# Packed values with v as weights, reciprocals through DRAM, and a new order of attention's steps

## Chip, core, metric

One core of one Trainium2 chip. The metric is the device time of one execution in microseconds (us), median of the runs. The profiled execution is one of its own, told beside them.

## The reference

The computation is attention through packed tokens, then two feed-forward networks, all in float32:

```
q, k, v: (8 batches, 8 heads, 576, 64);  p: (8, 8, 32, 64)
packed = softmax(p k^T / 8) v                 # per batch and head: 32 x 64
out    = softmax(q packed^T / 8) packed       # 576 x 64
x      = out as 4608 tokens x 512
x      = x / sqrt(mean(x^2) + 1e-6) * rms_g
x      = (silu(x w_gate) * (x w_val)) w_out   # 512 -> 1536 -> 512
h      = x w_in                               # 512 -> 2048
y      = (max(h, 0) + alpha * min(h, 0)) w_out2
```

Each softmax subtracts its row's maximum and adds 1e-9 to the sum of its exponentials.

## The kernel before

**Stages.** A prologue does batch 0's attention. Then come eight tiles, one for each batch's 576 tokens, in `tiles_of_a`; a tile has 24 blocks (`up_block`), each the gate and the value product of 128 hidden units and 288 tokens: 2 x 2 x 3 matmuls of 128x128 weights and 288 columns, "three passes" of float32 split in a high and a low part (L883 to L885). ScalarE takes the silu of the gate (L1373), VectorE the product with the value part (L1748). After the tiles, from about 423 us on apart from the last tile's blocks, come the wide products (`PHASES`); the change does not touch them.

**Attention beside the tiles.** While tile c - 1 runs, batch c's attention is done in its gaps ("batch c's share" below). Dictionaries give, for each engine, the names of the steps that stand at a place of a tile: `("within", i)` after the gate's part of block i (on VectorE and ScalarE: before their work on block i), `("ready", i)` before the last three matmuls of block i, `("after", i)` and then `("between", i)` behind it. `SECOND` holds batch 1's steps, `LATER` those of batches 2 to 7; `NEXT` the first steps of the batch behind (scores, maxima, exponentials, keys), `CARRIED` the last ones of the batch ahead (fold4, fold5). At one place, carried steps stand first, then the batch's own, then those of the next. The order on each engine is fixed by this; semaphores order the engines.

**The steps of a batch.** `scores` (p against k), their maxima and `exp`; `turn_keys`: VectorE transposes the exponentials in 32x32 blocks to `a_rows`, SP writes them to DRAM (`a_mid`) and `turned_keys` reads them back with keys in partitions (`a_keys`). `packed`: TensorE multiplies exponentials (weights, 128x32) by v (64 columns moving), VectorE scales rows by the reciprocal sums into `pp`, `turn_packed` transposes it on TensorE, ScalarE copies it to `pp_t`, and VectorE's `scaled` makes `pp_tg` (times `rms_g`). `tokens0/1`: scores of the 576 tokens against the packs, and the packs' own products. VectorE then works through `turn_s`, `max2`, `shift`, `sums`, `probs`, `turn_p` with ScalarE's exponentials between; `gram0/1` multiply the token weights by the packs' own products (`gram_sb`, 32x32 for each head), `weigh` and `means` give each token's mean square, `rsqrt` on ScalarE and `newton` on VectorE its inverse root, `normed` and `split` the scaled weights in two parts (`an_hi`, `an_lo`). `fold0` to `fold5` multiply the packed values by the gate and value weights (L1087), ScalarE casts the high part and VectorE subtracts the low part (`m_hi`, `m_lo`); these are the weights of the batch's tile.

**Waits that matter.** Block i's gate product may start when silu i - 2 is done, its value product when VectorE's product i - 2 is done (the two pairs of PSUM banks alternate). ScalarE loads a function table when it goes from silu to exponentials and back. `q_sb` lies on `k_sb`, so k of the next batch is loaded when this batch's tokens are done. SP's queue is in order: at each block stores of hidden units, moves of weight parts that GpSimd prepares in this stage, loads, and the two parts of `turn_keys`.

Of the kernel before, what the change touches and what calls it, by code (L numbers as in the profile page):

```python
# [7 lines left out]
F32 = mybir.dt.float32  # L8
# [5 lines left out]
P = 128  # L14
BATCH, HEADS, SEQ, HEAD_DIM = 8, 8, 576, 64
PACK = 32
# [49 lines left out]
           ("ready", 22): ["fold2_ready"], ("after", 22): ["fold2"],  # L66
# [8 lines left out]
            ("after", 20): ["newton"], ("within", 21): ["normed0"], ("after", 21): ["normed1", "fold1"],  # L75
            ("after", 22): ["split0"], ("within", 23): ["split1"], ("after", 23): ["fold2"],
            ("between", 23): ["fold3"]},
# [4 lines left out]
                   ("within", 22): ["split0"], ("after", 22): ["split1"], ("after", 23): ["fold2"], ("between", 23): ["fold3"]},  # L82
}
LATER = {
    "PE": {("between", 0): ["packed"], ("within", 2): ["turn_packed"],
           ("ready", 3): ["tokens0_ready"], ("after", 3): ["tokens0", "tokens1_ready", "tokens1"],
           ("between", 11): ["gram0", "fold0_ready", "fold0"],
           ("between", 13): ["gram1", "fold1_ready", "fold1"],
           ("between", 16): ["means", "fold2_ready", "fold2"],
           ("ready", 20): ["fold3_ready"], ("after", 20): ["fold3"]},  # L90
    "DVE": {("after", 0): ["norm0", "norm1", "packed"], ("after", 2): ["scaled"],
            ("after", 3): ["turn_s0", "gram"], ("after", 4): ["turn_s1", "max2_0"],
            ("after", 5): ["shift0", "max2_1"], ("within", 6): ["shift1"],
            ("between", 7): ["sums0"], ("after", 8): ["probs0"], ("after", 9): ["turn_p0", "sums1"],
            ("within", 10): ["probs1"], ("after", 10): ["turn_p1"],
            ("after", 11): ["weigh0"], ("after", 12): ["fold0"],
            ("after", 14): ["weigh1"], ("after", 15): ["fold1"],
            ("after", 17): ["newton"], ("after", 18): ["normed0"], ("after", 19): ["normed1", "fold2"],
            ("after", 20): ["split0"], ("after", 21): ["split1"], ("after", 22): ["fold3"]},
    "Activation": {("after", 2): ["packed"], ("after", 6): ["probs0", "probs1", "silu"], ("after", 12): ["fold0"],  # L100
                   ("after", 14): ["fold1"], ("after", 16): ["rsqrt"], ("after", 18): ["fold2"], ("after", 19): ["split0"],
# [4 lines left out]
    "DVE": {("between", 11): ["max0"], ("between", 13): ["max1"], ("between", 15): ["turn_keys"]},  # L106
# [87 lines left out]
def build(nc, q_t, k_t, v_s, p_t, w1_gv, w_parts, rms_g, alpha, out_t):  # L194
# [8 lines left out]
    with ExitStack() as ctx:  # L203
# [174 lines left out]
        def at_ps(c, t):  # L378
# [1633 lines left out]
```

## Time and profile before

| | |
|---|---|
| median of 3 runs | 1419.37 us (1418.79 to 1419.72) |
| profiled execution | 1417.08 us, span 1415.3 us |
| TensorE busy | 1391.8 us, 98% of the span |
| VectorE, ScalarE, GpSimd busy | 1067.0 (75%), 762.0 (54%), 271.1 us (19%) |
| granted TensorE clock | 0.999 of 2.4 GHz |
| busy share of the DMA engines | 80% |

"Busy" is the union of an engine's instructions. For TensorE their ends are modelled and overlap the next start, so short waits hide in it; the starts in the timeline tell more. Times in rows are from the span's start.

### The profile page before, as it was taken

The page shows a single profiled execution, that of the slowest core. Times are in us where ns is not written, and L with a number is a line of the kernel's source. Part 1 is how long each engine was busy: PE and PEld are TensorE (multiplying, and loading weights), DVE is VectorE, ACT ScalarE, POOL GpSimd, SP SyncE. Part 2 cuts the span into 40 slices and gives each one's busy share as a digit, 9 for nine tenths or more (in the row PEclk, how much of TensorE's full clock was granted, in tenths as well). Part 3 has the DMA queues.
Part 4 walks back from the last instruction along what each step waited for, and adds up shares of the span by engine and source line. Part 5 has one row for each costly group of instructions (what it writes and reads, how often), then busy time and mean ns, then how long its engine had stood idle before and what let it go on. Part 6 is the DMA issues. An engine that isn't in the chain of part 4 may idle for free.

```text
span 1415.3 us, 24525 instructions
## 1 busy us (share of the span) xinstructions
PE 1391.8 (98%) x9318; PEld 1194.7 (84%) x9318; DVE 1067.0 (75%) x1669; ACT 762.0 (54%) x1241; POOL 271.1 (19%) x464
## 2 busy tenths in 40 slices
PE   8999999999999999999999999999999999999998
PEld 4767787877879888888888888899888899999998
DVE  5767767777675689578987578986788876886786
ACT  4556466455543546356655356553566554664564
POOL 1744665666872000000000000000000000000000
PEclk9999999999999999999999999999999999999999
DMA  9768978979869987768797658798669788798775
GB/s 344 228 205 282 316 262 287 312 271 293 279 215 369 341 309 246 227 207 290 293 301 240 228 183 325 254 315 277 199 216 331 243 299 306 259 333 278 251 264 189
DMA packets 152372, 384.47 MB, mean 272 GB/s; under 512 B 9920, under 2 KB 66752, under 8 KB 143296
## 3 DMA queue, kind: packets, MB, share of 16 engines
q1 hardware_dynamic: 152112, 382.84, 80.0%
q8 instruction: 74, 1.21, 0.3%
q14 instruction: 42, 0.34, 0.1%
q10 hardware_dynamic: 144, 0.07, 0.0%
HBM read 286.27 MB, written 87.16 MB: 264 GB/s over the span
## 4 chain that ended last, share of the span: by engine, by line
PE 86%; DVE 5%; DMA 4%; ACT 3%; issue 2%; SPq 1%; POOL 0%; DVEq 0%; ACTq 0%; POOLq 0%
PE psum L883 27%; PE psum L884 27%; PE psum L885 27%; DMA k_sb<-k_t 3%; PE psum L1087 2%; PE psum L1028 1%; DVE act_sb L1748 1%; DMA g_sb<-rms_g 1%; PE psum L962 1%; PE psum L1049 0%; DVE m_lo L1690 0%; DVE sq L1657 0%; DVE sq L1654 0%; SPq L570 0%; ACT L1373 0%
## 5 line engine op out<-in xcount | busy, mean ns | idle before, releaser
L883 PE MATMUL psum<-stage_hi,ring 128*128 128x512 f32 (+1 forms) x980 | 360.3, 368 | 0.4
L885 PE MATMUL psum<-stage_lo,ring 128*128 128x512 f32 (+1 forms) x980 | 359.9, 367 | 0.0
L884 PE MATMUL psum<-stage_hi,ring 128*128 128x512 f32 (+1 forms) x980 | 359.9, 367 | 0.0
L1389 ACT CAST stage_hi<-g_sb 128x512 fp32r<-128x512 f32 (+1 forms) x384 | 221.9, 581 | 201.2 <-PE psum L885 198.6
L1767 DVE TENSOR_TENSOR stage_lo<-g_sb,stage_hi 128x512 fp32r<-128x512 f32 (+1 forms) x384 | 240.9, 638 | 67.4 <-ACT stage_hi L1389 66.6
L883 PE MATMUL psum<-an_hi,m_hi 128*128 128x288 f32 x768 | 236.0, 307 | 11.6 <-DVE act_sb L1748 5.9
L884 PE MATMUL psum<-an_hi,m_lo 128*128 128x288 f32 x768 | 226.1, 294 | 0.0
L885 PE MATMUL psum<-an_lo,m_hi 128*128 128x288 f32 x768 | 226.0, 294 | 0.0
L885 PE MATMUL psum<-x_lo,ring_up 128*128 128x512 f32 (+1 forms) x560 | 205.6, 367 | 0.0
L884 PE MATMUL psum<-x_hi,ring_up 128*128 128x512 f32 (+1 forms) x560 | 205.6, 367 | 0.0
L883 PE MATMUL psum<-x_hi,ring_up 128*128 128x512 f32 (+1 forms) x560 | 205.6, 367 | 0.0
L883 PEld LDWEIGHTS psum<-stage_hi,ring 128*128 128x128 f32 x980 | 184.0, 188 | 24.8 <-DVE stage_lo L1767 1.4
L885 PEld LDWEIGHTS psum<-stage_lo,ring 128*128 128x128 f32 x980 | 184.0, 188 | 22.9
L884 PEld LDWEIGHTS psum<-stage_hi,ring 128*128 128x128 f32 x980 | 184.0, 188 | 22.8
L883 PEld LDWEIGHTS psum<-an_hi,m_hi 128*128 128x128 f32 x768 | 144.2, 188 | 58.2 <-issue 33.0
L1748 DVE TENSOR_TENSOR act_sb<-act_sb,psum 128x288 f32<-128x288 f32 x192 | 85.6, 446 | 112.1 <-PE psum L885 60.0
L1373 ACT ACTIVATE act_sb<-psum 128x288 f32<-128x288 f32 x192 | 78.3, 413 | 152.4 <-PE psum L885 152.1
L884 PEld LDWEIGHTS psum<-an_hi,m_lo 128*128 128x128 f32 x768 | 144.6, 188 | 0.1
L885 PEld LDWEIGHTS psum<-an_lo,m_hi 128*128 128x128 f32 x768 | 144.4, 188 | 0.0
L885 PEld LDWEIGHTS psum<-x_lo,ring_up 128*128 128x128 f32 x560 | 105.1, 188 | 13.2
L883 PEld LDWEIGHTS psum<-x_hi,ring_up 128*128 128x128 f32 x560 | 105.1, 188 | 13.1
L884 PEld LDWEIGHTS psum<-x_hi,ring_up 128*128 128x128 f32 x560 | 105.1, 188 | 13.0
(152 smaller groups left out, 1775.2 us busy)
## 6 DMA issues: line engine op xcount, KB each, us to landing
ring<-w_down SPq DMA_DIRECT2D x70, 1024.0 KB, 5.2
ring<-w_out SPq DMA_DIRECT2D x70, 768.0 KB, 5.8
ring_up<-w_up SPq DMA_DIRECT2D x40, 1024.0 KB, 5.3
ring_up<-w_up SPq DMA_DIRECT2D x40, 768.0 KB, 4.6
h_mid<-act_sb SPq DMA_DIRECT2D x84, 288.0 KB, 4.2
g_sb<-h_mid SPq DMA_DIRECT2D x10, 1536.0 KB, 10.5
w_up<-parts SPq DMA_DIRECT2D x16, 896.0 KB, 5.9
w_down<-parts SPq DMA_DIRECT2D x16, 896.0 KB, 6.0
```

Of the source, the lines that this page charges most:

```text
L883: nc.tensor.matmul(dst, w_hi, hi, start=start, stop=False, skip_group_check=onto)
L884: nc.tensor.matmul(dst, w_lo, hi, start=False, stop=False, skip_group_check=onto)
L885: return nc.tensor.matmul(dst, w_hi, lo, start=False, stop=stop, skip_group_check=onto)
L962: mm = nc.tensor.matmul(pp_ps(c, e)[PACK * pair:PACK * (pair + 1), :], a_keys[:, e * PAIRS + pair, j, :], v_sb[:, j, head * HEAD_DIM:(head ...
L1028: mm = nc.tensor.matmul(psum[keys, gram_bank(c, h) + e, 0:HALF], gram_sb[keys, e, :], a2[keys, h, e, :], start=True, stop=True)
L1087: mm = nc.tensor.matmul(psum[keys, m_bank(c, j) + e, :].rearrange("p (f n) -> p f n", f=2), pp_tg[c % 2][dims, pair, :], gv_sb[dims, 2 * j ...
L1373: nc.scalar.activation(dst, gate_ps(n), ACT.Silu).then_inc(silu_done, 1)
L1389: nc.scalar.copy(stage_hi[:, n % STAGES, 0:w], block_of(k, ROLE[i], j)).then_inc(stage_hi_done, 1)
L1748: nc.vector.tensor_tensor(dst, dst, val_ps(n), ALU.mult).then_inc(h32_done, 1)
L1767: nc.vector.tensor_tensor(stage_lo[:, n % STAGES, 0:w], block_of(k, ROLE[i], j), stage_hi[:, n % STAGES, 0:w].bitcast(F32), ALU.subtract). ...
```

## The change

For batches 2 to 7, v's 64 dims of a head become the weights (128x64) and the exponentials move (32 columns), two heads side by side. The packed values come out turned, so `turn_packed` and ScalarE's copy go. The scaling must then be along columns: the reciprocal sums are written to DRAM and read back as a row for each pair, broadcast over 64 partitions (`rcp_rows`), and VectorE multiplies once. For all batches `gram_sb` becomes 128x128, zero outside the four heads' blocks by a mask (`own`) that GpSimd sets at the start, and `gram` is one matmul instead of four for each of its two halves. Many steps move by a block, k's load stands before and v's behind a part's moves, and some batches get dictionaries of their own.

```diff
@@ SECOND, batch 1 (only what changes) @@
-           ("ready", 22): ["fold2_ready"], ("after", 22): ["fold2"],
+           ("ready", 21): ["fold2_ready"], ("after", 21): ["fold2"],
...
-            ("after", 20): ["newton"], ("within", 21): ["normed0"], ("after", 21): ["normed1", "fold1"],
-            ("after", 22): ["split0"], ("within", 23): ["split1"], ("after", 23): ["fold2"],
-            ("between", 23): ["fold3"]},
+            ("within", 20): ["newton"], ("after", 20): ["normed0"], ("within", 21): ["normed1"], ("after", 21): ["fold1"],
+            ("within", 22): ["split0"], ("after", 22): ["split1", "fold2"], ("after", 23): ["fold3"]},
...
-                   ("within", 22): ["split0"], ("after", 22): ["split1"], ("after", 23): ["fold2"], ("between", 23): ["fold3"]},
+                   ("within", 21): ["split0"], ("after", 21): ["split1"], ("after", 22): ["fold2"], ("after", 23): ["fold3"]},
 LATER = {
-    "PE": {("between", 0): ["packed"], ("within", 2): ["turn_packed"],
+    "PE": {("between", 0): ["packed"],
            ("ready", 3): ["tokens0_ready"], ("after", 3): ["tokens0", "tokens1_ready", "tokens1"],
-           ("between", 11): ["gram0", "fold0_ready", "fold0"],
-           ("between", 13): ["gram1", "fold1_ready", "fold1"],
-           ("between", 16): ["means", "fold2_ready", "fold2"],
-           ("ready", 20): ["fold3_ready"], ("after", 20): ["fold3"]},
-    "DVE": {("after", 0): ["norm0", "norm1", "packed"], ("after", 2): ["scaled"],
+           ("between", 12): ["gram0", "fold0_ready", "fold0"],
+           ("between", 14): ["gram1", "fold1_ready", "fold1"],
+           ("between", 17): ["means", "fold2_ready", "fold2"],
+           ("between", 19): ["fold3_ready", "fold3"]},
+    "DVE": {("after", 0): ["packed", "scaled"],
             ("after", 3): ["turn_s0", "gram"], ("after", 4): ["turn_s1", "max2_0"],
             ("after", 5): ["shift0", "max2_1"], ("within", 6): ["shift1"],
-            ("between", 7): ["sums0"], ("after", 8): ["probs0"], ("after", 9): ["turn_p0", "sums1"],
-            ("within", 10): ["probs1"], ("after", 10): ["turn_p1"],
-            ("after", 11): ["weigh0"], ("after", 12): ["fold0"],
-            ("after", 14): ["weigh1"], ("after", 15): ["fold1"],
-            ("after", 17): ["newton"], ("after", 18): ["normed0"], ("after", 19): ["normed1", "fold2"],
+            ("between", 8): ["sums0"], ("after", 9): ["probs0"], ("after", 10): ["turn_p0", "sums1"],
+            ("within", 11): ["probs1"], ("after", 11): ["turn_p1"],
+            ("after", 12): ["weigh0"], ("after", 13): ["fold0"],
+            ("between", 15): ["fold1"], ("after", 15): ["weigh1"],
+            ("within", 18): ["newton"], ("after", 18): ["normed0"], ("after", 19): ["normed1", "fold2"],
             ("after", 20): ["split0"], ("after", 21): ["split1"], ("after", 22): ["fold3"]},
-    "Activation": {("after", 2): ["packed"], ("after", 6): ["probs0", "probs1", "silu"], ("after", 12): ["fold0"],
-                   ("after", 14): ["fold1"], ("after", 16): ["rsqrt"], ("after", 18): ["fold2"], ("after", 19): ["split0"],
+    "Activation": {("after", 7): ["probs0", "probs1", "silu"], ("after", 13): ["fold0"],
+                   ("after", 15): ["fold1"], ("after", 17): ["rsqrt"], ("after", 18): ["fold2"], ("after", 19): ["split0"],
                    ("after", 20): ["split1"], ("after", 21): ["fold3"]},
 }
...
-    "DVE": {("between", 11): ["max0"], ("between", 13): ["max1"], ("between", 15): ["turn_keys"]},
+    "DVE": {("between", 11): ["max0"], ("between", 13): ["max1"], ("between", 15): ["norm0", "norm1", "turn_keys"]},
...
+LAST_BATCH = {**LATER, "Activation": {**LATER["Activation"], ("after", 6): ["probs0", "probs1", "silu"], ("after", 7): []}}
+
+CARRIED_FIRST = {
+    "PE": {("ready", 6): ["fold4_ready", "fold5_ready"], ("after", 6): ["fold4", "fold5"]},
+    "DVE": {("between", 6): ["fold4"], ("after", 7): ["fold5"]},
+    "Activation": {("after", 6): ["fold4"], ("after", 7): ["fold5"]},
+}
+CARRIED_LAST = {
+    "PE": {("ready", 0): ["fold4_ready"], ("after", 0): ["fold4"], ("ready", 7): ["fold5_ready"], ("after", 7): ["fold5"]},
+    "DVE": {("after", 1): ["fold4"], ("after", 8): ["fold5"]},
+    "Activation": {("after", 1): ["fold4"], ("after", 8): ["fold5"]},
 }
...
-            return [4, 6, 4, 2, 6, 4][j] if first(c) else ([6, 6, 2, 6, 6, 6] if c == 1 else [6, 6, 6, 2, 6, 6])[j]
+            return [4, 6, 4, 2, 6, 4][j] if first(c) else ([6, 6, 2, 6, 6, 2] if c == 1 else [6, 6, 6, 2, 6, 6])[j]
...
             def turn_keys(c):
+                sp.wait_ge(rcp1_done, GROUPS * (c + 1))
+                reached(sp, rcp_in, 32 * (c - 2))
+                for g in range(GROUPS):
+                    sp.dma_start(rcp_mid[g].unsqueeze(1), rcp1[:, g:g + 1]).then_inc(rcp_out, 16)
                 for g in range(GROUPS):
                     sp.wait_ge(rows_turned, GROUPS * (c - 2) + g + 1)
                     sp.dma_start(a_mid[g], a_rows[:, g, :]).then_inc(rows_out, 16)
 
             def turned_keys(c):
                 sp.wait_ge(pp_mm, 2 * c)
+                sp.wait_ge(rcp_out, 16 * GROUPS * (c - 1))
+                sp.wait_ge(ppt_copied, c)
+                for e in range(2):
+                    sp.dma_start(rcp_rows[HEAD_DIM * e:HEAD_DIM * (e + 1)].rearrange("p q k -> p (q k)"),
+                                 rcp_mid[e].partition_broadcast(HEAD_DIM)).then_inc(rcp_in, 16)
                 sp.wait_ge(rows_out, 16 * GROUPS * (c - 1))
...
-                    if c + 1 < BATCH and i == (8 if c == 1 else 2):
+                    if c + 1 < BATCH and i == (8 if c == 1 else 7):
                         sp.wait_ge(pp_mm, 2 * c + 2)
                         load_v(c + 1)
-                    if c + 1 < BATCH and i == (10 if c == 1 else 4):
+                    if c + 1 < BATCH and i == (10 if c == 1 else 3):
...
+            nc.gpsimd.memset(own[:], 0.0).then_inc(zeroed, 1)
+            for pair in range(PAIRS):
+                pool.wait_ge(zeroed, pair + 2)
+                nc.gpsimd.memset(own[PACK * pair:PACK * (pair + 1), pair, :], 1.0).then_inc(zeroed, 1)
+            pool.wait_ge(zeroed, PAIRS + 2)
...
-                for e in range(2):
+                for pair in range(PAIRS):
                     for j in range(CHUNKS):
-                        for pair in range(PAIRS):
+                        for e in range(2):
                             head = 2 * pair + e
-                            mm = nc.tensor.matmul(pp_ps(c, e)[PACK * pair:PACK * (pair + 1), :],
+                            mm = nc.tensor.matmul(ppt_of(e)[:, PACK * pair:PACK * (pair + 1)],
+                                                  v_sb[:, j, head * HEAD_DIM:(head + 1) * HEAD_DIM],
                                                   a_keys[:, e * PAIRS + pair, j, :],
-                                                  v_sb[:, j, head * HEAD_DIM:(head + 1) * HEAD_DIM],
                                                   start=(j == 0), stop=(j == CHUNKS - 1))
-                    mm.then_inc(pp_mm, 1)
+                mm.then_inc(pp_mm, 2)
 
...
-                    for pair in range(PAIRS):
-                        keys = slice(PACK * pair, PACK * (pair + 1))
-                        mm = nc.tensor.matmul(psum[keys, gram_bank(c, h) + e, 0:HALF], gram_sb[keys, e, :], a2[keys, h, e, :],
-                                              start=True, stop=True)
+                    mm = nc.tensor.matmul(psum[:, gram_bank(c, h) + e, 0:HALF], gram_sb[:, e, :], a2[:, h, e, :],
+                                          start=True, stop=True)
...
             def norm(c, g):
 
                 n = GROUPS * c + g + 1
+                if g == 0:
+                    reached(dve, rcp_out, 16 * GROUPS * (c - 2))
                 dve.wait_ge(exp1_done, n)
...
             def packed(c):
+                if c > 1:
+                    dve.wait_ge(rcp_in, 32 * (c - 1))
+                    dve.wait_ge(pp_mm, 2 * c + 2)
+                    nc.vector.tensor_tensor(flat(pp_t[:]), psum[:, 3, 0:P], flat(rcp_rows[:]), ALU.mult).then_inc(ppt_copied, 1)
+                    return
                 reached(dve, ppt_mm, c)
                 dve.wait_ge(rcp1_done, 2 * c + 2)
                 for e in range(2):
             def scaled(c):
                 dve.wait_ge(ppt_copied, c + 1)
                 reached(dve, m_mm, NF1 // 2 * (c - 1))
-                nc.vector.tensor_tensor(pp_tg[c % 2][:], ppt_ps.rearrange("p (q k) -> p q k", q=PAIRS),
+                turned = pp_t[:] if c > 1 else ppt_ps.rearrange("p (q k) -> p q k", q=PAIRS)
+                nc.vector.tensor_tensor(pp_tg[c % 2][:], turned,
                                         g_sb[:].unsqueeze(2).to_broadcast([P, PAIRS, PACK]), ALU.mult).then_inc(ppg_done, 1)
 
...
-                bank, at = (4, 0) if first(c) else (2, HALF)
-                nc.vector.tensor_copy(gram_sb[:], psum[:, bank:bank + 2, at:at + PACK]).then_inc(gram_set, 2)
+                for e in range(2):
+                    within = own_ps(c, e).unsqueeze(1).to_broadcast([P, PAIRS, PACK])
+                    nc.vector.tensor_tensor(gram_sb[:, e, :].rearrange("p (q k) -> p q k", q=PAIRS), within, own[:],
+                                            ALU.mult).then_inc(gram_set, 1)
```

`CARRIED` itself stays; `SECOND`'s ScalarE steps split0 to fold3 come a block earlier. The new buffers are `own`, `rcp_rows` and `rcp_mid` (DRAM); `rinv_0` and `mean_0` move onto `a_keys`.

## Rows read from the trace of the kernel before

**Rows 1.** Who TensorE waited for, 97.5 to 423 us: idle in total, times, longest.

```profile
PE psum L883 <- DVE act_sb L1748: 4.6, 7, 1.6
PE psum L883 <- DMA k_sb<-k_t: 1.3, 3, 0.6
PE psum L1087 <- DVE m_lo L1690: 0.9, 2, 0.6
PE psum L883 <- DVE m_lo L1690: 0.7, 2, 0.3
PE psum L912 <- DMA k_sb<-k_t: 0.4, 2, 0.2
```

**Rows 2.** Timeline of TensorE, batch 5: start, duration, line, operands; packed step and transpose.

```profile
260.24 1.32 PE L962 MATMUL psum<-v_sb,a_keys 128*32 128x64 f32 x80
261.49 0.40 PE L883 MATMUL psum<-an_hi,m_hi 128*128 128x288 f32 x1
261.73 0.29 PE L884 MATMUL psum<-an_hi,m_lo 128*128 128x288 f32 x1
...
263.83 0.29 PE L885 MATMUL psum<-an_lo,m_hi 128*128 128x288 f32 x1
...
264.21 0.29 PE L884 MATMUL psum<-an_hi,m_lo 128*128 128x288 f32 x1
```

**Rows 3.** Timeline of TensorE, batch 5: a wait, gram0 and the means.

```profile
278.00 0.29 PE L885 MATMUL psum<-an_lo,m_hi 128*128 128x288 f32 x1
278.63 0.37 PE L883 MATMUL psum<-an_hi,m_hi 128*128 128x288 f32 x1 [0.34 <-DVE m_lo L1690]
...
284.03 1.17 PE L1028 MATMUL psum<-a,gram_sb 32*32 32x288 f32 x16
285.13 1.09 PE L1087 MATMUL psum<-gv_sb,pp_tg 64*32 64x512 f32 x16
...
296.47 1.13 PE L1049 MATMUL psum<-sq,mean_w 128*128 128x288 f32 x4
297.53 1.09 PE L1087 MATMUL psum<-gv_sb,pp_tg 64*32 64x512 f32 x16
```

**Rows 4.** Weight loads by shape, 97.5 to 423 us: busy us, mean ns.

```profile
L884 PEld LDWEIGHTS psum<-an_hi,m_lo 128*128 128x128 f32 x576 | 108.2, 188 | 0.0
...
L962 PEld LDWEIGHTS psum<-v_sb,a_keys 128*32 128x32 f32 x480 | 7.0, 110 | 5.0 <-issue 5.0
```

**Rows 5.** Timeline of ScalarE, batch 5: table, exponentials, silu, casts.

```profile
272.41 1.28 ACT L1290 ACT_TABLE_LOAD   x1
273.70 1.26 ACT L1292 ACTIVATE e<-e 128x576 f32<-128x576 f32 x2
...
276.28 0.41 ACT L1373 ACTIVATE act_sb<-psum 128x288 f32<-128x288 f32 x1
276.58 1.07 ACT L1335 CAST m_hi<-psum 128x512 fp32r<-128x512 f32 x2
...
290.55 0.77 ACT L1269 ACTIVATE a_sb<-a_sb,bias 128x576 f32<-128x576 f32 x1
```

**Rows 6.** Timeline of VectorE: row sums' start and second bias, batches 5 and 6.

```profile
278.40 0.74 DVE L1593 TENSOR_REDUCE sum<-e 128x18 f32<-128x576 f32 x1
...
290.93 0.15 DVE L1523 TENSOR_SCALAR bias<-negmax 128x1 f32<-128x1 f32 x1
...
332.46 0.74 DVE L1593 TENSOR_REDUCE sum<-e 128x18 f32<-128x576 f32 x1
...
345.94 0.15 DVE L1523 TENSOR_SCALAR bias<-negmax 128x1 f32<-128x1 f32 x1
```

**Rows 7.** Instructions on `a_keys`: first and last start; transfers' time to landing.

```profile
L962 PE MATMUL psum<-v_sb,a_keys x480: 218/219/244, 97.5 to 370.6; 128*32 128x64 f32 x160
L597 SPq DMA_DIRECT2D a_keys<-a_mid x24: 360/529/1384, 89.5 to 360.6; - x24
...
DMA to landing us min/median/max: 3.1/4.6/5.4
```

More of the change, by code:

```diff
@@ L111 @@
            ("ready", 15): ["scores1_ready"], ("after", 15): ["scores1"]},
-    "DVE": {("between", 16): ["max0", "max1"], ("between", 19): ["turn_keys"]},
+    "DVE": {("between", 16): ["max0", "max1"], ("between", 19): ["norm0", "norm1", "turn_keys"]},
     "Activation": {("after", 14): ["scores0"], ("between", 15): ["scores1"], ("after", 17): ["exp0", "exp1", "silu"]},
@@ L198, in build @@
     a_mid = nc.dram_tensor("a_mid", (GROUPS, P, SEQ), F32, kind="Internal").ap()
+    rcp_mid = nc.dram_tensor("rcp_mid", (GROUPS, P), F32, kind="Internal").ap()
     w_out = nc.dram_tensor("w_out", (PRODUCTS, P, DUOS1, 2, 2, P), F32, kind="Internal").ap()
@@ L250, in build @@
         a2 = place("a2", [P, 2, GROUPS, HALF])
-        gram_sb = place("gram_sb", [P, 2, PACK])
+        gram_sb = place("gram_sb", [P, 2, P])
+        own = place("own", [P, PAIRS, PACK])
         p_sb = place("p_sb", [P, PAIRS, PACK])
@@ L275, in build @@
         a_sb = place("a_sb", [P, GROUPS, SEQ])
+        a_keys_at = cursor[0]
         a_keys = place("a_keys", [P, HEADS, CHUNKS, PACK])
-        rinv_0, mean_0 = place("rinv_0", [P, 2, HALF]), place("mean_0", [P, 2, HALF])
-        assert gv_at + 4 * NF1 * KC * GV <= g_at + 4 * FIRST_CHUNK * 4 * WMAX and cursor[0] >= t3_at
+        assert gv_at + 4 * NF1 * KC * GV <= g_at + 4 * FIRST_CHUNK * 4 * WMAX
+        cursor[0] = max(cursor[0], t3_at)
         pp_tg = [place(f"pp_tg{n}", [P, PAIRS, PACK]) for n in range(2)]
+        rcp_rows = place("rcp_rows", [P, PAIRS, PACK])
+        rinv_0 = place("rinv_0", [P, 2, HALF], at=a_keys_at)
+        mean_0 = place("mean_0", [P, 2, HALF], at=a_keys_at + 2 * step)
         part_size, source_size = 4 * PRODUCTS * 2 * P, 4 * 4 * P
@@ L376, in pp_ps, with ppt_of @@
             return psum[:, e, 0:HEAD_DIM] if first(c) else psum[:, 3, e * HEAD_DIM:(e + 1) * HEAD_DIM]
+        def ppt_of(e):
+            return psum[HEAD_DIM * e:HEAD_DIM * (e + 1), 3, 0:P]
         def at_ps(c, t):
@@ L535, in at @@
                     place = (where, i)
-                    for name in (starting if c == 1 else CARRIED[name_of]).get(place, []):
+                    carried = (starting if c == 1 else CARRIED_FIRST[name_of] if c == 2 else
+                               CARRIED_LAST[name_of] if c == BATCH - 1 else CARRIED[name_of])
+                    for name in carried.get(place, []):
                         beside(c - 1, name)
                     if c < BATCH:
-                        for name in (SECOND if c == 1 else LATER)[name_of].get(place, []):
+                        steps = SECOND if c == 1 else LAST_BATCH if c == BATCH - 1 else LATER
+                        for name in steps[name_of].get(place, []):
                             beside(c, name)
@@ L982, in tokens_ready @@
                 else:
[L983 removed]
+                    pe.wait_ge(m_lo_done, evicted(c - 1) + 2 * (4 if c == 2 else 5))
             def tokens(c, h):
@@ L1072, in fold_ready @@
                     pe.wait_ge(m_lo_done, evicted(c) + 2 * 2)
+                elif j == 4 and c == 1:
+                    pe.wait_ge(s2_turned, 4 * (c + 1) + 4)
+                elif j == 5 and c == 1:
+                    pe.wait_ge(s2_turned, 4 * (c + 1) + 2)
+                    pe.wait_ge(gram_set, 2 * (c + 1) + 2)
                 elif j == 5 and c + 1 < BATCH:
```

3 lines of the change are left out of this document (2 added, 1 removed).

## Prediction

> **What bounds the kernel now.** I read the page first. TensorE counts as busy 98% of the span (the table ahead), so a stretch of the kernel costs what TensorE's own instructions cost there plus what it waits. The change touches only the stage with attention, to about 423 us; everything after it is left as it is.
>
> Busy time hides things here: a matmul's modelled end overlaps the next start. So I read starts. In batch 5's share of the stage (its packed step begins at 260.24, batch 6's at 314.29) 18 matmuls of the first matrix product lie between 261.49 and 263.83, 0.13 us each; a block of 12 is 1.58 us. Returning from small matmuls costs 0.11 more (261.49 to 261.73 is 0.24), and about 0.1 on the way out [rows 2].
>
> Then I read who makes TensorE wait. From 97.5 to 423 us it waits 16 times, 7.9 us by the view [rows 1]. By starts each is about 0.16 longer: at 278.00 the next start comes 0.63 later, 0.50 over the usual 0.13, where the view has 0.34 [rows 3]. That makes 7.9 + 16 x 0.16 = 10.5 us in six batches. Seven, 4.6 us, are for the product of block 18 or of another late block (L1748), held up by VectorE; the others are for k's transfer and for `m_lo`.
>
> **The change, part by part.** Times are against the profiled execution (1417.08 us, span 1415.3).
>
> *Packed values with v as weights.* Before: 40 calls, 80 instructions, weights 128x32 and 64 columns moving, four column tiles at once: 1.25 us to the next block [rows 2], or (1.25 - 0.11)/20 = 0.057 us for each four. After: 80 instructions with weights 128x64 and 32 columns moving, two tiles at once. Twice as many steps, 40. By the columns that move, each could take half: no change. By the weights, which are now twice as wide, it takes what their load takes. A load of 128 columns takes 188 ns and one of 32 takes 110 [rows 4]: 0.81 ns a column, so 64 columns stream in 52 ns (an estimate from the two rows). 40 x 0.052 + 0.11 = 2.19 us. That is +0.94 us, six times: **+5.6**. Bounds: 0 (loads hidden) and +12 (load and stream one after the other in each tile, 40 x (0.052 + 0.027) + 0.11 = 3.3). I take the load because 52 ns is above what 32 moving columns need (half of the 0.057 step) and the old step, where the load's 26 ns lay below, showed no sign of it.
>
> The Trainium skill, "TensorEngine Tiling (Array Packing)", section "Instruction Overhead", says that a matmul pays some 60 cycles, so that few moving columns cost as much as 60. By it 64 and 32 columns would cost alike, and this part would be 0; its 80 x 25 ns = 2.0 us (an estimate from the page) is contradicted by the 1.25 us for 80 instructions here.
>
> *No transpose of the packed values.* At 263.83 to 264.21 three starts take 0.38 instead of 0.26 [rows 2]: -0.12, six times: **-0.7**. ScalarE's copy and two VectorE scalings go, one VectorE product comes; none of them is waited for by TensorE.
>
> *Token weights as two full matmuls.* 1.10 us for 16 small ones (284.03 to 285.13) against 1.06 for the two full-size f32 calls of the means (296.47 to 297.53) [rows 3]: -0.04, some 15 times: **-0.6**. The masked copy is two VectorE products instead of one copy, some 0.3 us more. In batches 1 to 7 that lies in VectorE's idle time behind the transposes; in batch 0 the chain has no cover: **+0.3**. GpSimd's five small memsets end before the first data come.
>
> *Newton's step before block 18's product.* Now block 17's silu stands behind ScalarE's means chain, VectorE waits for it, then does Newton's three operations, then block 18's product, and block 20 waits. After the change the means stand after block 17, block 17's product is free of that chain, and fold3 (1.02 us) stands before block 20. Newton can start at the end of ScalarE's exponential, some 6.9 us after the means' start, and takes 2.3; block 20's second half starts 2 us later than that needs. So those waits go. k's load is issued ahead of a part's store and of v, so its waits go too, and m_lo's with it, since fold5's casts now stand ahead of the exponentials' table. I take all 16 as gone: **-10.5**.
>
> *What is late next.* Two things.
> (a) The exponentials now stand behind block 7's silu and behind fold5's two casts. From silu 7's start ScalarE does: 0.30 to the casts, casts 1.07, table 1.28, exponentials 1.26, table 1.28, silu 8 0.41 [rows 5], with gaps and the hand-over 5.7. Silu 7 starts 0.2 behind its gate. TensorE has from there: half a block 0.79, blocks 8 and 9 3.16, the scores' four passes (as the means', 1.06, plus 0.2) = 5.2. Block 10 needs silu 8: it waits 5.9 - 5.2 = 0.7 us, in the five batches that have scores: **+3.5**. Before, the exponentials stood one block earlier and the casts behind them.
> (b) With silu 8 late, VectorE's row sums ("between 8", behind block 8's product) start with block 10 at the earliest. From the sums to the second bias VectorE works without a pause: 278.40 to 291.08 = 12.7 us, and 13.6 in batch 6 [rows 6]; over the five batches 12.5 to 13.6, mean 12.9. The new order has the same work in that stretch. Behind the bias ScalarE needs the exponential (0.77 and its sum's read, 0.86), a table 1.28 and silu 14 0.41 [rows 5], together 2.65. TensorE needs silu 14 for block 16: six blocks 9.5 and two pairs of gram and fold (2 x (1.06 + 1.02 + 0.2)) after block 10's start, 14.1. Wait: 12.9 + 2.65 - 14.1 = 1.4 us, five times: **+7.1** (fold1's wait for fold0's `m_lo` is part of it). Bounds: 0 and 2.2 each.
>
> *Batch 1's end.* Newton, normed and fold2 come a block earlier and fold4 leaves the place before the packed step. That step began at 97.5 [rows 7] and could come at 93, but it needs the keys, whose transfers were issued from 89.5 and take up to 5.4 us to land, about 95 [rows 7]. Their issue can come 1 us earlier (block 21's product is earlier) and two more issues stand before them, so the keys still land at about 95. Gain 97.5 - 95.0 - 1.0 for fold4, which now follows: **-1.5** (bounds -3 and 0).
>
> *Reciprocals through DRAM.* Two writes of 128 values and two broadcasts, on SP's queue. At `i == 15` SP waits for VectorE's transposed rows in any case; the new wait for `rcp1_done` is earlier, since the norms stand directly before. Behind SP there stand block 15's store and a part's moves, which wait today too. The broadcasts stand before the four key transfers: they delay these, which take 4.6 us to land by the median [rows 7], by about 1, with some 2 us left before the packed step. **0** (without that cover, 1 us six times).
>
> Sum: 5.6 - 0.7 - 0.6 + 0.3 - 10.5 + 3.5 + 7.1 - 1.5 = +3.2, on a profiled 1417.1. The median of the runs shown is 2.3 above that execution; added to the median: 1419.4 + 3.2 = **1422.6 us**. What can be told from no change here is 0.2%, 2.8 us.
>
> **Rivals.**
> 1. *The packed step costs what it cost*, because weights are loaded behind the other tile's stream. For it: nothing in the old step shows a load. Against: 52 ns is longer than the stream. 1422.6 - 5.6 = 1417.0: within 0.2%. Chance 0.20.
> 2. *The two late silus don't stop TensorE* (faster). Place: blocks 10 and 16. It decides if silu 8 comes 0.7 us and silu 14 1.4 us sooner than I count, say if VectorE's chain is shorter because its long operations (1.4 us instead of 0.75 for one product of the same size) fall elsewhere. Against: the sequence on ScalarE is fixed and every length in it is steady. 1422.6 - 10.6 = 1412.0. Chance 0.23, since half of it would do for "faster" together with a cheaper packed step.
> 3. *Load and stream don't overlap within a tile.* 6 x (3.3 - 2.19) = 6.7 more: 1429.3. Against: the old step's 0.057 is less than 26 + 53. Chance 0.10. The Trainium skill, "TensorE: Matmul & The Clock Gate", section "The mechanism", says that a load overlaps a running matmul only where the row group differs, and both tiles here hold all rows; the old step, which is of the same kind, contradicts it by the sum just given.
> 4. *The keys are late* behind the reciprocals' transfers, in every batch: from 2 us on it decides; 1 us six times gives 1428.6. For it: the queue's work is in order. Chance 0.05.
>
> **How the numbers follow.** Forecast 0.42, its own range 1419.5 to 1427. It lies just over the 0.2% line (1422.2): about 0.33 of it slower, 0.09 same. Slower 0.33 + 0.10 + 0.05 less a little for batch 1's bound = 0.46; faster 0.23 and a few hundredths of rival 1 = 0.26; same 0.28. The range reaches from just above rival 2's full size to short of rival 3: 1412.5 to 1427.5.
>
> **What would show it.** The packed step (start of its first instruction to the next block's) at 2.2 us; no transpose behind it; no wait before block 20; in batches 2 to 6 a wait at block 10 that ScalarE's silu ends, about 0.7, and one at block 16, about 1.4, or at fold1 for `m_lo`; batch 5's period 1.3 longer than its 54.05 us; batch 7's some 1.7 shorter; the packed step of batch 2 near 95. Wrong it would be with a packed step of 1.3 or of 3.3, or with blocks 10 and 16 starting on time.

## The result, and the profile after

The changed kernel takes **1460.03 us** (median of 5 runs, 1458.47 to 1462.7), the kernel before 1419.72 us in the same comparison (1418.79 to 1420.55): ratio 1.0284, interval 1.027 to 1.0298. The forecast was 1422.6 with a range to 1427.5. The side was right, the size was not: 40 us instead of 3. The profiled execution has a span of 1458.2 us (before 1415.3), TensorE busy 1405.2 us, and a granted clock of 0.987.

The first view is again who TensorE waits for, from 97.5 us to the end of the tiles (engine, line <- what it waited for: us in total, times, longest):

```profile
PE psum L1002 <- DMA a_keys<-a_mid: 30.5, 6, 7.1
PE psum L923 <- ACT act_sb L1416: 7.0, 10, 0.8
PE psum L1130 <- DVE m_lo L1743: 0.5, 1, 0.5
PE psum L923 <- DVE act_sb L1801: 0.2, 1, 0.2
```

The waits of [rows 1] have gone almost all, as forecast. The ten for silu are (a) and (b) of the prediction. The first line is new: the packed step (L1002) waits for its keys in all six batches. The timeline of TensorE in batch 5 shows what such a wait does (start, duration, line, operands):

```profile
283.50 1.09 PE L1130 MATMUL psum<-gv_sb,pp_tg 64*32 64x512 f32 x16
289.59 4.48 PE L1002 MATMUL psum<-a_keys,v_sb 128*64 128x32 f32 x80 [5.00 <-DMA a_keys<-a_mid]
294.00 0.55 PE L923 MATMUL psum<-an_hi,m_hi 128*128 128x288 f32 x1
294.39 0.30 PE L924 MATMUL psum<-an_hi,m_lo 128*128 128x288 f32 x1
```

From the step's start to the next block are 4.41 us, against 1.25 in [rows 2] and 2.19 forecast. The table by windows explains it (start:end, length, busy us and instructions of PE, PEld, DVE, ACT and POOL, granted clock, DMA share, GB/s):

```profile
281.00:284.00 3.00, 3.00 (x36) 2.51 (x34) 1.87 (x4) 0.82 (x2) 0.00 (x0) 1.00 1.00 406
284.60:289.50 4.90, 0.00 (x0) 0.00 (x0) 0.00 (x0) 0.00 (x0) 2.85 (x7) 0.80 1.16 295
289.60:293.90 4.30, 4.30 (x80) 4.30 (x80) 0.00 (x0) 0.00 (x0) 3.21 (x6) 0.50 1.04 417
294.50:298.00 3.50, 3.50 (x29) 3.50 (x28) 2.33 (x5) 1.79 (x4) 3.44 (x7) 1.00 0.48 189
```

TensorE stood idle for 5 us, the granted clock fell in that time from 1.00 to 0.50 (2.4 to 1.2 GHz), and the whole packed step ran at the lower level.

Why the keys are late stands in SP's waits (97.5 to 505) and in its timeline:

```profile
SPq L617 <- DVE rcp L1578: 38.0, 5, 8.2
SPq L625 <- DMA rcp_mid<-rcp: 22.3, 5, 5.6
```

```profile
269.51 0.80 SPq L617 DMA_DIRECT2D rcp_mid<-rcp  x2
270.35 0.90 SPq L620 DMA_DIRECT2D a_mid<-a_rows  x2
...
279.19 2.39 SPq L627 DMA_DIRECT2D rcp_rows<-rcp_mid  x2
281.62 2.08 SPq L632 DMA_DIRECT2D a_keys<-a_mid  x4
```

The wait at L617 is for VectorE and harmless: SP has arrived early. The one at L625 isn't: SP stands until 1 KB of reciprocals, issued at 269.5, is in DRAM, and goes on at 279.2. The keys are issued at 281.6, 11.3 us behind the rows. The transfers of that stretch (269.5 to 281; the digits are the busy share of the 16 DMA engines in 40 equal slices, below them the GB/s moved):

```profile
DMA  0002207999999090013969999219990176921099
GB/s 0 0 0 2 2 0 305 385 385 369 321 16 16 0 8 0 0 8 24 32 24 40 24 56 16 16 16 97 40 32 16 16 24 72 88 16 24 16 361 483
```

From the twelfth slice to the 38th (272.7 to 280.4) the DMA engines are busy half of the time (5.1 tenths, the mean of the digits) and move 27 GB/s (mean of the figures), where just before and after that they move 300 to 480. Busy share without throughput: something is stuck in front.

### The profile page after: what moved, and what is told of

The parts are those of the page before. It is cut to its first block, busy times and chain, and to the rows that moved or that the text cites. A ratio compares the mean times of both kernels' runs of the same rounds, so it can differ in the third digit from the quotient of the medians.

```text
span 1458.2 us, 24157 instructions
## 1 busy us (share of the span) xinstructions
PE 1405.2 (96%) x9120; PEld 1217.8 (84%) x9120; DVE 1065.1 (73%) x1671; ACT 760.1 (52%) x1235; POOL 261.6 (18%) x469
## 4 chain that ended last, share of the span: by engine, by line
PE 80%; DVE 7%; DMA 7%; ACT 3%; issue 2%; SPq 1%; POOL 0%; DVEq 0%; ACTq 0%; POOLq 0%
PE psum L923 25%; PE psum L924 25%; PE psum L925 25%; DMA a_keys<-a_mid 2%; DMA a_mid<-a_rows 2%; DMA rcp_mid<-rcp 2%; PE psum L1002 2%; PE psum L1130 1%; DVE act_sb L1801 1%; DVE m_lo L1743 1%; ACT L1405 1%; SPq L632 1%; DVE sq L1684 1%; PE psum L1032 0%; DVE a L1662 0%
## 5 line engine op out<-in xcount | busy, mean ns | idle before, releaser
L923 PE MATMUL psum<-an_hi,m_hi 128*128 128x288 f32 x768 | 235.6, 307 | 10.6 <-ACT act_sb L1416 7.9
## 6 DMA issues: line engine op xcount, KB each, us to landing
g_sb<-h_mid SPq DMA_DIRECT2D x10, 1536.0 KB, 10.5
```

Of the source, the lines that this page charges most:

```text
L923: nc.tensor.matmul(dst, w_hi, hi, start=start, stop=False, skip_group_check=onto)
```

## The experiments

### First: which part of the change costs what

**The new order alone** (old packed step, reciprocals used in SBUF as before, full-size token weights kept):

```diff
@@ in words @@
-    a_keys moving, v as weights; rcp_mid written and read; L1002's loop
+    v moving, a_keys as weights, turn_packed, scaling of rows: as in the kernel before
```

> The new order and the full-size gram stay, packed values and reciprocals are as before the change (exponentials as weights, transpose, two scalings, no transfer of reciprocals). Theory 1 (the loss is the packed step, 6 x 3.2 = 19 us, and the waits for the keys behind the reciprocals' transfers, 6 x 5 = 30 us; the order by itself gains): 1460 - 49 = about 1411, faster than before by 8. Theory 2 (the new order, with v's load behind, makes the keys late): still waits of about 5 us before the packed step, about 1441.

Measured 1412.66 us (1411.27 to 1413.16), ratio 0.9938, interval 0.9916 to 0.9961. The packed step is back to 1.25 us and its keys are late once, by 1.1. So the new order is a gain of 8.8 us by the medians (5.8 us by the profiled executions), and the whole loss of the change lies in the packed step and the way of its inputs.

**The new packed step, reciprocals kept in SBUF.** VectorE scales the exponentials' rows before it transposes them; nothing goes through DRAM that did not before:

```diff
+    nc.vector.tensor_scalar(a_sb[:, g, :], a_sb[:, g, :], rcp1[:, g:g + 1], None, ALU.mult)
     nc.vector.transpose(a_rows[:, g, :], a_sb[:, g, :])
-    sp.dma_start(rcp_mid...), sp.dma_start(rcp_rows...)
```

> As after the change, but VectorE scales the exponentials by the reciprocal sums before it transposes them (two more operations of 128x576 a batch), and no reciprocal goes through DRAM. Theory 1: the keys land some 9 us after the rows' store instead of 19, no wait before the packed step, the packed step stays at 4.4 us: 1460 - 30 = about 1430. Theory 2: waits stay, 1455 or more.

Measured 1422.38 us (1421.24 to 1423.52), ratio 1.0007, interval 0.9994 to 1.002: no difference from before that can be told. I had expected some 1430, with a packed step that stays at 4.4 us. It doesn't: with its inputs in time it runs at the full clock and takes 2.46 us in all six batches:

```profile
264.54 2.52 PE L993 MATMUL psum<-a_keys,v_sb 128*64 128x32 f32 x80
266.99 0.40 PE L914 MATMUL psum<-an_hi,m_hi 128*128 128x288 f32 x1
```

That is +1.21 each and +7.3 in all; with 3.5 us more waits for VectorE's products, and 0.7 less for the transposes that are gone, it is 10.1, and the medians are 9.7 us over the order alone.

**Rows and keys ahead of the reciprocals** in SP's queue, all else as in the changed kernel:

```diff
@@ in words @@
+    rows' write, then the reciprocals' write; keys' read, then the reciprocals' read
-    the other way round
```

> As after the change, but the rows' store is issued ahead of the reciprocals' write, and the keys' load ahead of the reciprocals' read. If what costs is only that rows and keys stand behind the small transfers in the queue: no wait before the packed step, about 1430. If the small writes hold up all that shares the 16 engines, wherever they stand: the keys are still late, or VectorE's product waits for the reciprocals, and the time stays over 1440.

Measured 1455.99 us (1454.76 to 1461.46), ratio 1.0249, interval 1.0222 to 1.0277. The keys are as late as before (30.1 us in all). The rows, now in front, land 2.3 us after their issue by the median, though single ones still take up to 11. But the keys' transfers, issued from 209.6 in batch 4 while SP need not wait for the reciprocals, take 12 to 13 us to land (6.6 by the median of all batches, 4.5 in the order alone). The place in front isn't enough: what is issued behind the reciprocals' write is slow.

**Both moves added to the kernel before**, with their result unused:

```diff
+    sp.dma_start(rcp_mid[g].unsqueeze(1), rcp1[:, g:g + 1])       # ahead of the rows
+    sp.dma_start(rcp_rows[...], rcp_mid[e].partition_broadcast(HEAD_DIM))  # ahead of the keys
```

> The kernel before, with the reciprocals' write and read added at the same places of SP's queue (and the norms moved ahead of the keys' transposes); nobody uses what is read. Theory 1: the keys land some 8 us later than before, the packed step waits about 4 us in each of six batches: about 1443. Theory 2: within 0.3% of before.

Measured 1439.17 us (1438.59 to 1441.04), ratio 1.0126, interval 1.0106 to 1.0146: about 18 us of the loss, in the old order too. The keys there are late by 15.4 us in all.

### Second: the write or the read, the bytes or the place

All of these but the last stand on the new order alone (1412.7 us), and nobody reads the values.

**The write alone, and the same with each value 512 bytes from the next:**

```diff
+    sp.dma_start(rcp_mid[g].unsqueeze(1), rcp1[:, g:g + 1])      # rcp_mid (2, 128)
```
```diff
+    sp.dma_start(rcp_mid[g, :, 0:1], rcp1[:, g:g + 1])           # rcp_mid (2, 128, 128)
```

> The new order with the old packed step (1412.7 us), and only the two writes of 128 reciprocals of 4 bytes, which nobody reads. Theory W (the writes themselves hold the transfer queue): the rows behind them land some 10 us after their issue instead of 2.1, the keys' issue waits for that, the packed step waits 3 to 5 us in five or six batches at once with a fall of the clock: 1430 to 1440. Theory R (the broadcasts hold it): 1412 to 1415 and rows that land in 2 to 3 us.

> As the run before, but every one of the 256 values goes to an address 512 bytes from the next. If the writes are slow because all of them fall into the same few hundred bytes of DRAM, the rows land in 2 to 4 us and the time is 1412 to 1416. If they are slow because each is a transfer of 4 bytes, nothing changes against the run before (1430 to 1440).

The write alone: 1443.31 us (1442.3 to 1446.47), ratio 1.017, interval 1.0154 to 1.0186. It costs 30.6 us. That is somewhat above the 1430 to 1440 expected. The same 256 values of 4 bytes, spread: 1411.54 us (1410.94 to 1412.41), ratio 0.9943, interval 0.9928 to 0.9957: nothing. SP's timeline, first side by side, then apart:

```profile
198.77 0.79 SPq L617 DMA_DIRECT2D rcp_mid<-rcp  x2
199.61 0.91 SPq L620 DMA_DIRECT2D a_mid<-a_rows  x2
209.62 1.89 SPq L627 DMA_DIRECT2D a_keys<-a_mid  x4
```

```profile
188.63 0.80 SPq L617 DMA_DIRECT2D rcp_mid<-rcp  x2
189.47 0.91 SPq L620 DMA_DIRECT2D a_mid<-a_rows  x2
193.53 3.29 SPq L627 DMA_DIRECT2D a_keys<-a_mid  x4
```

The issues of writes and rows cost SP the same. From the rows' issue to the keys' are 10 us against 4.1. Side by side, SP stands there until the rows are in DRAM, as its waits say; apart, that line is gone, the writes land in 1.5 us by the median and the rows in 2.5:

```profile
SPq L624 <- DMA a_mid<-a_rows: 27.2, 5, 6.3
```

**The read alone** (the write made for batch 2 only):

```diff
+    if c == 2: sp.dma_start(rcp_mid[g].unsqueeze(1), rcp1[:, g:g + 1])
+    sp.dma_start(rcp_rows[...], rcp_mid[e].partition_broadcast(HEAD_DIM))   # every batch
```

> As the first, but the reciprocals are written for batch 2 alone and the two broadcasts over 64 partitions are made in every batch (unused). Theory W: the keys land 1 to 2 us later than in the new order alone, about 6.5 us after their issue, and the packed step waits little: 1413 to 1420. Theory R: 1430 to 1440.

Measured 1419.0 us (1417.44 to 1423.47), ratio 1.0005, interval 0.9992 to 1.0017. The only late keys are batch 2's, behind the one write, by 5.1 us, and there the packed step runs at half clock (2.29 us), as does the block behind it until 103.6. Wait, step and block account for the 6.3 us over the order alone. From batch 3 on the broadcasts cost TensorE nothing: the packed step starts on time.

**The changed kernel, reciprocals turned first.** VectorE transposes them in 32x32 blocks, so that a write is 4 runs of 128 bytes:

```diff
+    nc.vector.tensor_copy(rcp_wide[:, 0:GROUPS], rcp1[:])
+    nc.vector.transpose(rcp_turned[:], rcp_wide[:])
-    sp.dma_start(rcp_mid[g].unsqueeze(1), rcp1[:, g:g + 1])
+    sp.dma_start(rcp_mid[g].rearrange("(q k) -> q k", k=PACK), rcp_turned[g:P:PACK, :])
```

> The changed kernel with one thing different: VectorE turns the reciprocals in 32x32 blocks first, so each write is 4 runs of 128 bytes instead of 128 values of 4 bytes. If the number of small pieces holds the queue, the writes and the rows land in 2 to 3 us, the keys are late by 0 to 1 us a batch, the packed step takes 2.46 us at the full clock, and the time is 1418 to 1425 (1422.4 with the reciprocals kept in SBUF, less 4 us of VectorE waits there). If any extra transfer and its wait in SP's queue is enough, the keys still wait 4 to 5 us a batch: 1450 to 1460.

Measured 1420.95 us (1418.95 to 1424.56), ratio 1.0008, interval 0.9996 to 1.002. With the same waits, the same queue and the same bytes, 39 of the 40 us are gone. The packed step takes 2.46 us, and only batch 2's keys are late, by 2.3.

### Third: the packed step, and the silu waits

**Three forms of the packed step** on the kernel with reciprocals kept in SBUF (one execution each, read from the traces): the five calls of a head in a row instead of alternating between the heads; each moving column given twice; and 32 dims as weights in four column tiles.

```diff
-    for j in range(CHUNKS):
-        for e in range(2):
+    for e in range(2):
+        for j in range(CHUNKS):
```
```diff
-    a_keys[:, e * PAIRS + pair, j, :]
+    a_keys[:, e * PAIRS + pair, j, :].unsqueeze(1).to_broadcast([P, 2, PACK])
```
```diff
-    for e in range(2):      # weights v_sb[:, j, 64 dims of head 2 * pair + e]
+    for n in range(4):      # weights v_sb[:, j, 32 dims], output psum[32 * n:32 * (n + 1)]
```

> The changed kernel with reciprocals kept in SBUF (its packed step took 2.46 us at the full clock), the five calls of one head one after the other instead of alternating between the two halves of TensorE's columns. If the overlap needs neighbours in different halves the step takes 3.5 to 4.8 us, otherwise 2.46.

> As the run before in its base, with every one of the 32 moving columns given twice, so 64 columns move past the same weights. If the weights' load sets the step (my forecast: two halves side by side, 59 ns a pair of instructions) it stays 2.46 us. If load and stream lie one behind the other in each half (old step 57 ns for 32 + 64 columns, new step 59 ns for 64 + 32: 0.6 ns a column), it takes 40 x 0.078 + 0.11 = 3.2 us.

> The same base with 32 of a head's dims as weights in each call, four column tiles side by side, 160 instructions instead of 80. Load alone: 40 x 0.026 + 0.11 = 1.15 us; load and stream one after the other: 40 x 0.038 + 0.11 = 1.65 us; if each instruction costs what it costs now (31 ns) however narrow it is: 4.9 us.

In that order, the step and the block behind it:

```profile
266.81 3.41 PE L993 MATMUL psum<-a_keys,v_sb 128*64 128x32 f32 x80
270.15 0.40 PE L914 MATMUL psum<-an_hi,m_hi 128*128 128x288 f32 x1
```
```profile
263.22 2.55 PE L994 MATMUL psum<-a_keys,v_sb 128*64 128x64 f32 x80
265.71 0.40 PE L914 MATMUL psum<-an_hi,m_hi 128*128 128x288 f32 x1
```
```profile
266.38 1.56 PE L993 MATMUL psum<-a_keys,v_sb 128*32 128x32 f32 x160
267.88 0.40 PE L914 MATMUL psum<-an_hi,m_hi 128*128 128x288 f32 x1
```

The executions took 1427.65, 1423.07 and 1438.31 us. Start to start the steps take 3.33, 2.48 and 1.49 us; only the second is one of the values expected. Less the 0.11 for the switch and divided by the rounds (one instruction in each tile that runs side by side), weights x moving columns:

| form | tiles | rounds | ns a round |
|---|---|---|---|
| before: 32 x 64 | 4 | 20 | 57 |
| changed: 64 x 32 | 2 | 40 | 59 |
| moving columns doubled: 64 x 64 | 2 | 40 | 59 |
| 32 x 32 | 4 | 40 | 34.5 |

Twice the moving columns cost nothing, half the weights' width saves 24 ns. In these four forms, whose neighbouring instructions go to different tiles, a round takes what the wider of load and stream takes, about 0.9 ns a column at 64. That the sum of both counts is refuted by the third line (78 ns expected, 59 measured). The form with a head's calls in a row has 40 ns an instruction against 29.5 in the alternating one. It doesn't follow from this reading as it stands: a tile that takes 59 ns for its load would take 59, not 40, unless the other tile's instructions still ran beside it for part of the time. The runs don't tell which, so the reading is shown for the alternating forms alone.

The third form's step is 0.97 us shorter than its base's, yet its execution is 16 us longer: TensorE has five waits in it, 15.0 us in all, that no semaphore ends:

```profile
PE psum L914 <- issue: 6.9, 2, 4.4
PE psum L916 <- issue: 4.4, 2, 3.0
PE psum L993 <- issue: 3.7, 1, 3.7
```

The edit adds 80 matmul instructions to a batch, and as many weight loads. The DMA view has a queue of the kind "instruction", which brings pieces of 16 KB. Each of the five waits has just one such piece in it or at its start, and TensorE goes on 1.4 to 1.6 us after the piece has ended. For the longest wait, the view from 331 to 332.2 and the end of the wait:

```profile
q8 instruction: 1, 0.02, 5.0%
```
```profile
333.55 0.61 PE L914 MATMUL psum<-an_hi,m_hi 128*128 128x288 f32 x1 [4.42 <-issue]
```

So TensorE most likely ran out of instructions behind a step that uses them up in 1.5 us. This is read from the trace; no run varied it.

**The token exponentials a block earlier**, on the new order alone:

```diff
-    "Activation": {..., ("after", 7): ["probs0", "probs1", "silu"]
+    "Activation": {..., ("after", 6): ["probs0", "probs1", "silu"]
```

> The new order with the old packed step (1412.7 us), with the token exponentials of batches 2 to 7 back behind block 6's silu. My theory: both waits of TensorE for silu (blocks 10 and 16, 0.8 us each, 7.2 in all) come from the exponentials' late place; they go, and the time is 1412.7 - 7 = 1405 to 1407. The rival: the old place brings back the waits that the old order had (for m_lo and VectorE's products), and the time is 1410 to 1414.

Measured 1409.16 us (1408.46 to 1409.72), ratio 0.992, interval 0.9906 to 0.9934: the lowest median of all versions. It gains 3.5 us over the order alone by the medians and 2.1 by the profiled spans (1409.5 and 1407.4), where I expected some 7. The two intervals (to 0.9934, and from 0.9916) overlap a little. Its waits:

```profile
PE psum L914 <- ACT act_sb L1407: 2.9, 4, 1.3
PE psum L914 <- DVE m_lo L1726: 1.9, 5, 0.4
PE psum L993 <- DMA a_keys<-a_mid: 1.0, 1, 1.0
```

Silu's waits fall from 7.2 us (ten) to 2.9 (four), and five for `m_lo` appear, 1.9 us (the kernel before had four, 1.6 us; the order alone has one, 0.8): both theories have a part.

### Fourth: how near, and two terms of the sum

**The unused write with 64, and with 16 bytes between the values** (one execution each):

```diff
-    rcp_mid (GROUPS, P, P)
+    rcp_mid (GROUPS, P, 16)        # and in the other run (GROUPS, P, 4)
```

> The new order with the unused write of the reciprocals, each value 64 bytes from the next (at 4 bytes apart: rows land 9 us after their issue, 1443; at 512 apart: 2.2 us, 1411.5). If small writes are held up only when they fall in one piece of 64 bytes or less, this is as at 512: rows in 2.2 us, 1410 to 1413. If the piece is 512 bytes: between the two, rows in 3 to 9 us, 1415 to 1443.

> As the run before with 16 bytes between the values. If writes within 64 bytes of each other hold each other up, four values share a piece instead of 16: the writes still take a good part of their 7 us, rows in 3 to 7 us, 1412 to 1435. If the piece is 16 bytes or less, 1410 to 1413.

1411.01 and 1412.29 us. The rows' time to landing, first at 64 bytes, then at 16 (minimum, median, maximum; at 512 it was 2.2/2.5/4.8):

```profile
DMA to landing us min/median/max: 2.2/2.5/5.8
```
```profile
DMA to landing us min/median/max: 3.1/3.3/6.5
```

At 64 bytes there is nothing left of the effect; at 16, four values to each 64 bytes, the rows are 0.8 us later; at 4 bytes, sixteen to each, they land 9 to 10 us after their issue. The cost grows with the number of small writes that fall close together. At 16 it came out at the lower end of what I had expected.

**Small token weights again**, on the new order alone:

```diff
-    gram_sb (128, 2, 128), one matmul a half, masked by own
+    gram_sb (128, 2, 32), four matmuls a half, one copy
```

> The new order (1412.7 us) with the packs' own products as four small matmuls a half and one copy, as before. By my terms (-0.6 and +0.3 for the full-size version) this is 0.3 us slower: 1412.5 to 1413.5. If the mask on VectorE costs anything in batches 1 to 7, it is faster by 1 or more: 1409 to 1412.

Measured 1412.48 us (1412.1 to 1414.04), ratio 0.9953, interval 0.994 to 0.9967, against 0.9938 (0.9916 to 0.9961) with the full-size ones. The intervals overlap: that part of the change is worth nothing that can be told.

**VectorE's sums and probabilities a block earlier too:**

```diff
-    ("between", 8): ["sums0"], ("after", 9): ["probs0"], ("after", 10): ["turn_p0", "sums1"], ("within", 11): ["probs1"], ("after", 11): ["turn_p1"]
+    ("between", 7): ["sums0"], ("after", 8): ["probs0"], ("after", 9): ["turn_p0", "sums1"], ("within", 10): ["probs1"], ("after", 10): ["turn_p1"]
```

> As the run with the token exponentials a block earlier (1409.2 us), and VectorE's sums, probabilities and transposes a block earlier too, where they stood before. VectorE then fills the 1.3 us that it is idle in block 9, its second maximum comes earlier, and block 16's wait for the silu (2.9 us over four places) goes: 1405 to 1407. Rival: the sums now stand in front of a product that TensorE waits for, and the time is 1409 to 1413.

Measured 1415.46 us (1414.23 to 1417.4), ratio 0.9975, interval 0.9966 to 0.9984: 6.3 slower than without it, and above both values expected. The waits for silu fall to 1.6 us, but the sums now stand in front of products that TensorE needs:

```profile
PE psum L914 <- DVE act_sb L1784: 4.1, 6, 1.7
PE psum L914 <- DVE m_lo L1726: 2.1, 5, 0.4
PE psum L914 <- ACT act_sb L1407: 1.6, 2, 1.3
```

With the 1.2 us for batch 2's keys, TensorE waits some 3 us longer here than in the version before, and the profiled spans (1413.0 and 1407.4) are 5.6 apart: the rest isn't placed.

## Why the prediction was wrong

**The step that failed** is "Reciprocals through DRAM ... 0". It gave the two writes no time of their own, and looked for cover at the broadcasts. The write costs 30.6 us by itself; the read costs nothing once the write is out of the way, and in the changed kernel 39 of the 40 us go when the write leaves in runs. The sentence "the new wait for `rcp1_done` is earlier" looked at the wrong wait: not the one for the values to be ready, but those for values and rows to be in DRAM (L625 and the one ahead of L632), which hold SP's queue. In batch 5 the keys are issued 11.3 us behind the rows; in the new order alone it is 5.1. Slack was about what was said: 2.9 us there between the keys' landing (254.8) and the packed step (257.7). With it used up, the wait is 5.0. Rival 4 named the place and the sign, and set its price at 1 us a batch and its chance at 0.05: the old trace has no transfer of 4-byte pieces, and the prediction went by large ones, without a bound for pieces some 500 times smaller. Its condition, "from 2 us on it decides", was met in every batch.

**What was missing altogether** is the clock. A late input was priced at its lateness. The six waits are 29.7 us longer by starts than in the new order alone (33.7 against 4.0, from the start before the packed step to its own). The packed steps add 17.8 more: 25.3 us in the six batches against 7.5, of which 7.3 are their price at the full clock and 10.5 the halved one. 29.7 + 17.8 = 47.5. The profiled spans are 48.7 apart (the medians 47.4): the blocks right behind the steps, whose starts are 0.24 us apart instead of 0.13 until the clock is back, add some 2, and the transposes that are gone take 0.7 off. The Trainium skill, "TensorE: Matmul & The Clock Gate", section "HAM oscillation — how this bites in real kernels", describes a clock that falls while TensorE waits for DMA, so that the next work starts at the lower level; the windows above agree (1.00 to 0.50 in 5 us of idle time).

**The side was luck.** Forecast and result are both slower, but not for the same reason. With the reciprocals in runs the change costs 1.0 us (ratio 1.0008, interval 0.9996 to 1.002), which can't be told from nothing: the term that was put at 0 made the whole difference. That this is near the +3.2 of the sum is luck too, since two errors cancel. The new order gained 5.8 us by the profiled executions (8.8 by the medians) and not 1.7, and the new packed step with the reciprocals in runs cost 8.3 us over the order alone by the medians (9.3 by the spans), where the sum has 4.9 for packed step and transpose.

**The other terms:**
- *Packed step +5.6*: +7.3 measured (2.46 us instead of 2.19). The choice of the load over the stream was right; the column costs 0.92 ns and not 0.81. Rival 3 (3.3 us) and rival 1 (1.25) are refuted. The Trainium skill, "TensorEngine Tiling (Array Packing)", section "Instruction Overhead", puts each matmul at some 60 cycles, 25 ns at 2.4 GHz (an estimate from the page), and one with few moving columns at as much as one with 60. The runs differ: 160 instructions took 1.49 us, 9 ns each, and with 32 moving columns a round took 59 or 34.5 ns by the width of the weights.
- *Sixteen waits gone, -10.5*: right but for 0.7 us in two places (0.8 in one in the order alone).
- *(a) 0.7 us at block 10*: right, 0.77 by the view, 0.85 by starts. *(b) 1.4 us at block 16*: 0.56 to 0.86 by starts, mean 0.78, so the chain from the sums to silu 14 is 0.6 shorter than I made it (0.1 of that is my sum: 0.86, 1.28 and 0.41 are 2.55, not 2.65). Together 5 x 0.85 + 5 x 0.78 = 8.2 instead of 10.6. Rival 2 (no waits) is refuted.
- *Batch 1's end -1.5*: the packed step of batch 2 starts at 95.06 in the new order alone instead of 97.54: -2.5.
- *Gram -0.6 and +0.3*: nothing that can be told.

Without the packed step the terms make -1.7 for the new order. Its profiled execution is 5.8 us shorter than that of before (spans 1409.5 and 1415.3), so my sum is 4.1 short: 2.4 of it in the silu waits, 1.0 in batch 1, and 0.7 that I can't place. By the medians the gain is 8.8, and 3 more stay unplaced.

## What to carry to other kernels

Don't write a column of one 4-byte value per partition to neighbouring addresses in DRAM in a stretch where other transfers have a deadline: turn it first, so that it leaves in runs, or spread it. Price a small transfer by what is queued behind it and behind the wait for it, not by its bytes, and look in the DMA view for engines that are busy and move little. And where TensorE gets a wait of several us, count with the stretch behind it at half the clock.

## What was not expected of the hardware

- 256 writes of 4 bytes side by side held the DMA engines for some 8 us, in which 27 GB/s moved instead of 300 and more; with 16 bytes or more between them they landed in 1.5 us by the median. The Trainium skill, "DMA: Bandwidth & Descriptors", section "Specifications", says that below 512 bytes a transfer becomes a read-modify-write. The size alone doesn't explain these runs, as the pieces had 4 bytes in the fast ones too; read-modify-writes of the same small piece of DRAM that wait for each other would, but the runs show only that nearness counts.
- Whether and when the clock falls doesn't go by the length of the wait. With both moves added to the kernel before, TensorE waited before all its packed steps. After 2.69 us of idle time the step took 2.29 us, at a granted clock of 0.50. After 3.83 it took 1.34, since the clock fell only in its course, and after 3.03 it took 1.25 and the clock didn't fall at all:

```profile
155.77 1.42 PE L974 MATMUL psum<-v_sb,a_keys 128*32 128x64 f32 x80 [3.83 <-DMA a_keys<-a_mid]
...
273.49 2.36 PE L974 MATMUL psum<-v_sb,a_keys 128*32 128x64 f32 x80 [2.69 <-DMA a_keys<-a_mid]
...
332.39 1.32 PE L974 MATMUL psum<-v_sb,a_keys 128*32 128x64 f32 x80 [3.03 <-DMA a_keys<-a_mid]
```

- With 80 more matmul instructions a batch, five waits of up to 4.4 us appeared, 15 us in all, that no semaphore ends. In each, TensorE goes on 1.4 to 1.6 us after a 16 KB piece on the "instruction" queue has ended.
